# First-layer products of the prologue in fp32, key step on POOL

## The chip, the cores and the metric

The kernel runs on one core of a Trainium2 chip. The metric is the device time of one execution in microseconds; lower is better. Before the change it is 1369.68 us, the median of three runs (1369.66 to 1371.54).

The engines of a core work side by side, each through its own list of instructions in order: PE (TensorE, matrix products, from SBUF into PSUM), DVE (VectorE), ACT (ScalarE), POOL (GpSimd), and SP (SyncE), which here only issues transfers. They meet at semaphores.

## The reference

Three stages follow one another. The first is a gated linear attention over 768 steps for 4 x 8 heads of 48; the second a mixture of four experts, all of them applied, weighed by normalised probabilities; the third a gated two-layer network.

```python
for t in range(S):
    state = alpha[:, :, t, :, None] * state + k[t] (outer) v[t]
    y[:, :, t] = q[t] @ state
x = y as rows of 3072 tokens by 384
p = domain_probs / domain_probs.sum(-1)
out = sum over e of p[:, e] * (relu(x @ w1[e]) @ w2[e])      # 4 experts, 384 -> 1024 -> 384
h = out @ w_in                                               # 384 -> 2048
result = (h * clip(h + 3, 0, 6) / 6) @ w_out                 # 2048 -> 384
```

All inputs and outputs are fp32.

## The kernel before, in words

**Tiles.** The 3072 tokens make 6 tiles of 512. Attention is done in chunks of 64 steps for all heads, 8 chunks to a tile (`PER_TILE`). The two networks are cut into slots: a slot is 128 hidden units, its weights are 384 columns for the first layer and 384 for the second (128x768 together). A tile has 32 slots of the experts and 16 of the third stage.

**Products in two parts.** A product of fp32 operands in the networks is made of three products in a reduced format (fp32r): each operand is split into a high part (a rounded copy, made by ACT) and a low part (the rest). `hidden(g)` is the first layer of slot g (L571 to L589): for each of three blocks of x (`K3`) the products hi*hi, hi*lo and lo*hi, at L587. `project(g)` is the second layer (L591 to L607, product at L606). `weights_hi(g)` (L951 to L955, ACT) and `weights_lo(g)` (L1069 to L1077, POOL) split a slot's weights from the loaded `w_raw`, a ring of 4, into the rings `w_hi` and `w_lo` of 8.

**Attention of a chunk n.** POOL makes the decays and scales k level by level (`scale_k`, steps 0 to 5; the step into `k_top` is L1053). The last step, into `k_level(n, 6)`, is made by ACT for the first eight chunks (`scale_k_last`, L883 to L890, four copies) and by POOL from chunk 8 on (L1048). DVE scales q (`scale_q`, L664 and L680). PE makes the scores (`score`, L498), turns the keys (`turn_k`, L510), and does `attend`: masked scores by v (L540), the new part of the state (`carry`, L520), and q by the state (L555). Between `score` and `attend` DVE masks the scores (`keep`, L697 and L709), with two of the levels copied by ACT (`copy_high`, L905). After `attend` DVE forms the next state (L721) and turns y (L727), ACT writes the high part of x (`split_x`, L930), and DVE the low part (L733). `score(n+2)` writes the PSUM banks that y(n) was in, and so waits for these two parts.

**The prologue.** The first tile's eight chunks are done before the main loop over slots. PE's order is: score(n+1), a warming matmul on zeros (`keep_warm`, L563, 128x256 in fp32), attend(n), turn_k(n+1), and after chunks 4, 5 and 6 two early slots each (`early_after`): the first layer of slots 0 to 5 for the first half of the tile's tokens, the 256 of chunks 0 to 3 (`HALF`). After the early slots 4 and 5 come five warming matmuls, attend(7), four more, and the main loop with slot 0. There, slots 0 to 5 do the second half of the tokens only. ACT splits high parts of slots 0 to 5 in its iterations 0 to 5; POOL low parts of slots 0 to 5 in its iterations 3 to 8 of ten, right after its first k step, in two halves.

**The main loop.** For every slot g PE does `hidden(g)`, then `score`, `turn_k` or `attend` of a chunk of the next tile where tables place them, then `project(g - 2)`. Weights are split three slots ahead and loaded six ahead. SP's queue holds all loads in one order, so a load that waits holds those behind it.

## Time and profile before

| | before |
|---|---|
| median of three runs | 1369.68 us |
| profiled execution | 1370.62 us |
| its span | 1368.8 us |
| PE busy | 1349.2 us (99%) |
| POOL busy | 781.8 us (57%) |
| DVE busy | 653.9 us (48%) |
| ACT busy | 553.6 us (40%) |
| granted PE clock, mean | 0.999 |

The span is the time from the first to the last instruction in the profile; the execution has 1.8 us around it. Busy shares are means over the span. The chain that ended last goes back from the last instruction, at each step to what released it, or to the instruction before it on its engine.

### The profile page before, as it was taken

The numbers are of one execution on the slowest core, as the hardware profiler recorded it, in microseconds if no ns is written. First come the engines' busy times: TensorE is split into PE (matmuls) and PEld (weight loads), VectorE is DVE, ScalarE is ACT, GpSimd is POOL, SyncE is SP. The second block draws the span as 40 slices with busy tenths as digits, with TensorE's granted clock in tenths as the row PEclk, the third lists the DMA queues.
The fourth block names the chain that finished last, engine by engine and source line by source line (L and its number), as shares of the span: only waits on it lengthen the run. The fifth ranks groups of instructions, "written<-read, shape, count | busy, mean of one in ns | idle before, by whom it ended". The sixth has DMA issues, their size and how long they took to land.

```text
span 1368.8 us, 34311 instructions
## 1 busy us (share of the span) xinstructions
PE 1349.2 (99%) x13638; PEld 1104.4 (81%) x13638; DVE 653.9 (48%) x1382; ACT 553.6 (40%) x1078; POOL 781.8 (57%) x862
## 2 busy tenths in 40 slices
PE   7899999999999999999999999999999999999998
PEld 5788888888888888888888888888888888888887
DVE  7756655444544544454544444444445333333333
ACT  5633333333444333355332345433335433335543
POOL 8956665566556565656556555665564444444442
PEclk9999999999999999999999999999999999999999
DMA  5353333333333433333433333343332343323331
GB/s 161 91 169 111 110 110 117 109 117 98 100 123 104 141 99 125 96 107 108 149 105 107 108 107 106 117 129 112 98 97 85 98 127 103 110 93 93 103 116 35
DMA packets 76045, 150.35 MB, mean 110 GB/s; under 512 B 8816, under 2 KB 33648, under 8 KB 75888
## 3 DMA queue, kind: packets, MB, share of 16 engines
q1 hardware_dynamic: 75888, 148.16, 34.2%
q8 instruction: 111, 1.82, 0.6%
q14 instruction: 46, 0.38, 0.1%
HBM read 143.36 MB, written 4.77 MB: 108 GB/s over the span
## 4 chain that ended last, share of the span: by engine, by line
PE 97%; DVE 1%; issue 1%; POOL 0%; DMA 0%; ACT 0%; DVEq 0%; POOLq 0%
PE psum L606 44%; PE psum L587 43%; PE psum L498 5%; PE psum L520 1%; PE psum L540 1%; PE psum L555 1%; PE psum L510 1%; PE psum L563 1%; DMA alpha_q<-qa 0%; DVE q_lev L680 0%; POOL k_lev L1057 0%; DVE result L780 0%; DVE alpha_q L680 0%; DVE alpha_q L664 0%; DVE decay L651 0%
## 5 line engine op out<-in xcount | busy, mean ns | idle before, releaser
L1076 POOL TENSOR_TENSOR w_lo<-w_raw,w_hi 128x768 fp32r<-128x768 f32 (+1 forms) x294 | 532.7, 1813 | 538.4 <-ACT w_hi L955 538.1
L948 ACT ACTIVATE h_hi<-psum 128x512 fp32r<-128x512 f32 (+1 forms) x288 | 171.1, 595 | 613.9 <-DVE psum L741 531.3
L606 PE MATMUL psum<-h_hi,w_hi 128*128 128x512 f32 x855 | 341.0, 399 | 0.2 <-DVE x_lo L776 0.2
L587 PE MATMUL psum<-x_hi,w_hi 128*128 128x512 f32 (+1 forms) x882 | 339.8, 385 | 0.4 <-issue 0.4
L587 PE MATMUL psum<-x_lo,w_hi 128*128 128x512 f32 (+1 forms) x882 | 339.3, 385 | 0.0
L587 PE MATMUL psum<-x_hi,w_lo 128*128 128x512 f32 (+1 forms) x882 | 339.2, 385 | 0.0
L606 PE MATMUL psum<-h_hi,w_lo 128*128 128x512 f32 x855 | 333.7, 390 | 0.0
L606 PE MATMUL psum<-h_lo,w_hi 128*128 128x512 f32 x855 | 333.2, 390 | 0.0
L741 DVE SCALAR_TENSOR_TENSOR psum<-psum,probs 128x512 f32<-128x512 f32 x184 | 128.6, 699 | 353.4 <-PE psum L587 353.3
L955 ACT ACTIVATE w_hi<-w_raw 128x768 fp32r<-128x768 f32 x288 | 241.5, 838 | 0.1
L759 DVE TENSOR_TENSOR h_lo<-psum,h_hi 128x512 fp32r<-128x512 f32 x280 | 192.3, 687 | 61.0 <-ACT h_hi L948 61.0
L587 PEld LDWEIGHTS psum<-x_hi,w_hi 128*128 128x128 f32 x882 | 165.7, 188 | 34.0 <-issue 0.7
L587 PEld LDWEIGHTS psum<-x_hi,w_lo 128*128 128x128 f32 x882 | 165.7, 188 | 33.2
L587 PEld LDWEIGHTS psum<-x_lo,w_hi 128*128 128x128 f32 x882 | 165.7, 188 | 33.1
L606 PEld LDWEIGHTS psum<-h_hi,w_lo 128*128 128x128 f32 x855 | 160.5, 188 | 34.4
L606 PEld LDWEIGHTS psum<-h_hi,w_hi 128*128 128x128 f32 x855 | 160.5, 188 | 34.2 <-issue 0.6
L606 PEld LDWEIGHTS psum<-h_lo,w_hi 128*128 128x128 f32 x855 | 160.7, 188 | 31.1
L747 DVE SCALAR_TENSOR_TENSOR psum<-gate,psum 128x512 f32<-128x512 f32 x96 | 66.8, 696 | 198.7 <-ACT gate L936 198.7
L936 ACT ACTIVATE gate<-psum,three 128x512 f32<-128x512 f32 x96 | 66.3, 691 | 141.6 <-PE psum L587 141.6
L1057 POOL TENSOR_TENSOR k_lev<-k_lev,decay 128x256 f32<-128x256 f32 x144 | 96.0, 667 | 6.8 <-ACT k_lev L880 0.5
L709 DVE COPY_PREDICATED p_kept<-level_sb,psum 128x128 f32<-128x128 int32 x224 | 74.0, 330 | 5.6
L1020 POOL TENSOR_TENSOR decay<-decay 128x64 f32<-128x64 f32 (+3 forms) x184 | 58.7, 319 | 11.9
(71 smaller groups left out, 843.1 us busy)
## 6 DMA issues: line engine op xcount, KB each, us to landing
w_raw<-w SPq DMA_DIRECT2D x288, 384.0 KB, 3.0
alpha_q<-qa SPq DMA_DIRECT2D x48, 256.0 KB, 3.7
k_raw<-kk SPq DMA_DIRECT2D x48, 128.0 KB, 3.5
probs<-prob_scratch SPq DMA_DIRECT2D x24, 256.0 KB, 3.9
v_sb<-v SPq DMA_DIRECT2D x48, 96.0 KB, 3.0
out<-result SPq DMA_DIRECT2D x18, 256.0 KB, 3.9
level_sb<-level SPq DMA_DIRECT2D x1, 80.0 KB, 3.0
ident_sb<-ident SPq DMA_DIRECT2D x1, 64.0 KB, 3.2
```

Source lines behind the costliest of these rows:

```text
L498: mm = pe.matmul(j_out[own(jj), lo:lo + width], k_level(n, l)[own(i), j, :], moving, start=True, stop=True)
L587: mm = pe.matmul(h_bank[g % 2][:, cols], a, x[:, cols], start=k == 0 and i == 0, stop=k == K3 - 1 and i == 2)
L606: mm = pe.matmul(out_bank[k], a, x, start=first and i == 0, stop=(last or g == PLAIN - 1) and i == 2, skip_group_check=ph == 0)
L709: dve.copy_predicated(dst.rearrange("p a (m r x) -> p a m r x", r=2, x=x)[:, :, :, 1, :], mask, s[:, :, at:at + CH // 2].rearrange("p a (m ...
L741: dve.scalar_tensor_tensor(out=h_bank[g % 2][:, :], in0=h_bank[g % 2][:, :], scalar=0.0, in1=probs[:, t % 2, u, :], op0=ALU.max, op1=ALU.m ...
L747: dve.scalar_tensor_tensor(out=h_bank[g % 2][:, :], in0=gate[:, g % 2, :], scalar=6.0, in1=h_bank[g % 2][:, :], op0=ALU.min, op1=ALU.mult) ...
L759: op = dve.tensor_tensor(lo, h_bank[g % 2][:, :], hi, ALU.subtract)
L936: act.activation(gate[:, g % 2, :], h_bank[g % 2][:, :], ACT.Relu, bias=three[:, :]).then_inc(gate_made, 1)
L948: act.activation(h_at(h_hi, x_hi, g)[:, cols], h_bank[g % 2][:, cols], ACT.Relu if g < PLAIN else ACT.Copy).then_inc(hh_made, 1)
L955: act.activation(w_hi[:, g % RING, :], w_raw[:, g % RAW, :], ACT.Copy).then_inc(w_hi_made, 1)
L1057: op = pool.tensor_tensor(b, a, dec.to_broadcast([P, m, 2, x]), ALU.mult)
L1076: op = pool.tensor_tensor(w_lo[:, g % RING, cols], w_raw[:, g % RAW, cols], w_hi[:, g % RING, cols].bitcast(F32), ALU.subtract)
```

## The change

The first layer of the six early slots is no longer done with three reduced products per block, but with one fp32 product per block (`hidden_early`), straight from the loaded weights `w_raw` and from a copy of x in fp32. ACT writes that copy (`keep_x`) for chunks 0 to 3 into `result`, a tile that the prologue doesn't use otherwise. The ring of raw weights is freed for slots 4 and 5 only when the early slot that read it is done (`h_made` in `load_w`), and these two loads stand one iteration later in SP's order. The last key step of the first eight chunks goes from ACT to POOL. In the prologue ACT and POOL split the weights of slots 0 to 4 instead of 0 to 5; POOL does it in its iterations 5 to 9; slot 5 is split in the main loop, at slot 2. `EARLY` stays 6, so the two new loops over `early_after(PER_TILE - 1)` are empty.

```diff
--- before.py
+++ after.py
@@ -40,7 +40,8 @@
 DEEP = 3
 BEHIND = 2
 PLAIN = FT
-EARLY = 6
+EARLY = 2 * DEEP
+SPLIT_EARLY = 5
 EARLY_FROM = PER_TILE // 2
 HALF = TILE // 2
 SPLIT_AHEAD = 3
@@ -52,7 +53,6 @@
 Z_STEPS = LEVELS - 1
 Z_FIRST = 2
 K_STEPS = 6
-K_SCALES = 4
 KEEPS = LEVELS
 HIGHS = 6
 K_TOP = PAIRS * CH + CH // 2
@@ -143,11 +143,6 @@
 
 def last_of_seq(n):
     return n % SEQ_CH == SEQ_CH - 1
-
-
-def scaled(n):
-
-    return K_STEPS * n - min(n, PER_TILE)
 
 
 def keeps(n):
@@ -236,7 +231,7 @@
         in_prob_rows, prob_rows_out, prob_made = sem("in_prob_rows"), sem("prob_rows_out"), sem("prob_made")
         zeros_made, ones_made, p_zeroed = sem("zeros_made"), sem("ones_made"), sem("p_zeroed")
         three_made = sem("three_made")
-        q_made, k_made, k_last_made = sem("q_made"), sem("k_made"), sem("k_last_made")
+        q_made, k_made = sem("q_made"), sem("k_made")
         z_made, z_first_made, total_made = sem("z_made"), sem("z_first_made"), sem("total_made")
         k_odd_made = sem("k_odd_made")
         p_made, kt_made = sem("p_made"), sem("kt_made")
@@ -244,7 +239,7 @@
         keep_made, high_made, kn_made, dec_made, s_made = sem("keep_made"), sem("high_made"), sem("kn_made"), sem("dec_made"), sem("s_made")
         yt_made, x_hi_made, x_lo_made = sem("yt_made"), sem("x_hi_made"), sem("x_lo_made")
         w_hi_made, w_lo_made = sem("w_hi_made"), sem("w_lo_made")
-        h_made, gate_made, h_out, out_weighed = sem("h_made"), sem("gate_made"), sem("h_out"), sem("out_weighed")
+        h_made, gate_made, h_out, out_weighed, x_kept_made = sem("h_made"), sem("gate_made"), sem("h_out"), sem("out_weighed"), sem("x_kept_made")
         hh_made, hl_made = sem("hh_made"), sem("hl_made")
         out_made, x2_hi_made, out_free = sem("out_made"), sem("x2_hi_made"), sem("out_free")
         stored = sem("stored")
@@ -404,6 +399,7 @@
 
                 need(sp, w_hi_made, g - RAW + 1)
                 need(sp, w_lo_made, g - RAW + 1)
+                need(sp, h_made, min(g - RAW + 1, EARLY))
                 u = PHASE_OF[g]
                 f = g - STARTS[u] + (0 if PHASES[u][0] == "E" else E_SLOTS)
                 sp.dma_start(w_raw[:, g % RAW, :], w[f]).then_inc(in_w[g % RAW], 16)
@@ -436,12 +432,12 @@
                 load_qk(n + QRING)
                 if n > 0:
                     load_v(n + 1)
-                if RAW <= n < LOAD_AHEAD:
-                    load_w(n)
+                if RAW < n <= EARLY:
+                    load_w(n - 1)
             load_v(PER_TILE + 1)
             sp.dma_start(prob_rows[:, :, :], dp.rearrange("e (p n) -> p e n", p=P)).then_inc(in_prob_rows, 16)
             for g in range(SLOTS):
-                if g + LOAD_AHEAD < SLOTS:
+                if EARLY <= g + LOAD_AHEAD < SLOTS:
                     load_w(g + LOAD_AHEAD)
                 if g in SCORE_AT and SCORE_AT[g] + QRING < CHUNKS:
                     load_qk(SCORE_AT[g] + QRING)
@@ -476,7 +472,7 @@
                 pe.wait_ge(in_k[n % QRING], 16 * (n // QRING + 1))
                 pe.wait_ge(k_odd_made, n + 1)
                 pe.wait_ge(q_made, Q_STEPS * n + LEVELS)
-                pe.wait_ge(k_made, scaled(n) + LEVELS - 1)
+                pe.wait_ge(k_made, K_STEPS * n + LEVELS - 1)
                 for l in range(LEVELS):
                     at, width = ((0, CH // 2), (CH // 2, CH))[l] if l < 2 else (CH // 2 * (l + 1), CH // 2)
                     for jp in range(2):
@@ -503,8 +499,7 @@
 
                 if n == 0:
                     pe.wait_ge(in_ident, 16)
-                pe.wait_ge(k_made, scaled(n + 1))
-                pe.wait_ge(k_last_made, K_SCALES * min(n + 1, PER_TILE))
+                pe.wait_ge(k_made, K_STEPS * (n + 1))
                 need(pe, kn_made, carried(n))
                 for jp in range(2):
                     mm = pe.transpose(kt_out[:, jp * P:(jp + 1) * P], k_level(n, LEVELS)[:, 2 * jp:2 * jp + 2, :],
@@ -562,22 +557,30 @@
                 for _ in range(n):
                     pe.matmul(out_bank[2][:, 0:2 * P], zeros_sb[:, 0:P], zeros_sb[:, :], start=True, stop=True)
 
-            def hidden(g, early=False):
+            def hidden_early(g):
+
+                pe.wait_ge(x_kept_made, EARLY_FROM)
+                need(pe, hh_made, made(g, early=True) - 2)
+                need(pe, hl_made, made(g, early=True) - 2)
+                pe.wait_ge(in_w[g % RAW], 16 * (g // RAW + 1))
+                for k in range(K3):
+                    mm = pe.matmul(h_bank[g % 2][:, 0:HALF], w_raw[:, g % RAW, k * P:(k + 1) * P], result[:, k, 0:HALF],
+                                   start=k == 0, stop=k == K3 - 1)
+                mm.then_inc(h_made, 1)
+
+            def hidden(g):
 
                 kind, t = PHASES[PHASE_OF[g]]
-                first = g == STARTS[PHASE_OF[g]] and not early
-                cols = columns_of(g, early)
-                if early:
-                    pe.wait_ge(x_hi_made, EARLY_FROM)
-                    pe.wait_ge(x_lo_made, EARLY_FROM)
+                first = g == STARTS[PHASE_OF[g]]
+                cols = columns_of(g)
                 if first and kind == "E":
                     pe.wait_ge(x_hi_made, PER_TILE * (t + 1))
                     pe.wait_ge(x_lo_made, PER_TILE * (t + 1))
                 if first and kind == "M":
                     pe.wait_ge(x2_hi_made, K3 * (t + 1))
                     pe.wait_ge(out_free, K3 * (PHASES.index(("E", t)) + 1))
-                need(pe, hh_made, made(g, early) - 2)
-                need(pe, hl_made, made(g, early) - 2)
+                pe.wait_ge(hh_made, made(g) - 2)
+                pe.wait_ge(hl_made, made(g) - 2)
                 pe.wait_ge(w_hi_made, g + 1)
                 pe.wait_ge(w_lo_made, g + 1)
                 for k in range(K3):
@@ -623,7 +626,7 @@
                     if not early_after(n):
                         keep_warm(1)
                 for g in early_after(n):
-                    hidden(g, early=True)
+                    hidden_early(g)
             for g in range(SLOTS):
                 hidden(g)
                 if g in SCORE_AT:
@@ -837,6 +840,8 @@
                 split_x(n)
                 if not last:
                     scale_q(ahead, at + behind + 1)
+            for g in early_after(PER_TILE - 1):
+                hidden_lo(g, early=True)
             for step in range(Q_EARLY):
                 scale_q(Q_BEFORE, step)
             for g in range(SLOTS):
@@ -879,16 +884,6 @@
                 a, b = (k_level(n, l).rearrange("p j (m r) -> p j m r", r=2)[:, :, :, 1] for l in (0, 1))
                 act.activation(b, a, ACT.Copy).then_inc(k_odd_made, 1)
 
-            def scale_k_last(n):
-
-                wait_decays(act, n, LEVELS - 1)
-                act.wait_ge(k_made, scaled(n) + LEVELS - 1)
-                need(act, kt_made, carried(n - 1))
-                dec = decay_k(n, LEVELS - 1)
-                for j in range(PAIRS):
-                    act.activation(k_level(n, LEVELS)[:, j, 0:CH // 2], k_level(n, LEVELS - 1)[:, j, 0:CH // 2],
-                                   ACT.Copy, scale=dec[:, j, 0:1]).then_inc(k_last_made, 1)
-
             def copy_high(n):
 
                 s = scores(n)[:, :].rearrange("p (a c) -> p a c", c=SLAB)
@@ -919,6 +914,13 @@
                     act.activation(state_decayed[:, j, :], state[n % 2][:, j, :], ACT.Copy,
                                    scale=total[n % 2][:, j:j + 1]).then_inc(dec_made, 1)
 
+            def keep_x(n):
+
+                act.wait_ge(yt_made, n + 1)
+                cols = slice(n * CH, (n + 1) * CH)
+                act.activation(result[:, :, cols].rearrange("p b (h t) -> p b h t", h=2), y_blocks(n), ACT.Copy
+                               ).then_inc(x_kept_made, 1)
+
             def split_x(n):
 
                 t = n // PER_TILE
@@ -966,9 +968,7 @@
             odd_k(0)
             odd_k(1)
             odd_k(2)
-            scale_k_last(0)
             copy_high(0)
-            scale_k_last(1)
             for n in range(PER_TILE):
                 copy_k_rows(n)
                 for g in early_after(n - 1):
@@ -979,11 +979,13 @@
                     odd_k(n + 3)
                 if n + 1 < PER_TILE:
                     copy_high(n + 1)
-                if n < EARLY:
+                if n < SPLIT_EARLY:
                     weights_hi(n)
+                if n < EARLY_FROM:
+                    keep_x(n)
                 split_x(n)
-                if n + 2 < PER_TILE:
-                    scale_k_last(n + 2)
+            for g in early_after(PER_TILE - 1):
+                hidden_hi(g, early=True)
             for g in range(SLOTS):
                 if g > BEHIND and g - BEHIND in STARTS and PHASES[PHASE_OF[g - BEHIND - 1]][0] == "E":
                     x2_hi(PHASE_OF[g - BEHIND - 1])
@@ -992,7 +994,7 @@
                 hidden_hi(g)
                 if g in STATE_AT:
                     split_x(STATE_AT[g])
-                if EARLY <= g + SPLIT_AHEAD < SLOTS:
+                if SPLIT_EARLY <= g + SPLIT_AHEAD < SLOTS:
                     weights_hi(g + SPLIT_AHEAD)
                 if g in SCORE_AT:
                     n = SCORE_AT[g]
@@ -1014,8 +1016,6 @@
                     need(pool, q_made, Q_STEPS * (n - 1))
                 else:
                     wait_decays(pool, n, l - 1)
-                if l == LEVELS - 1:
-                    need(pool, k_last_made, K_SCALES * min(n - 1, PER_TILE))
                 first, second = decay_operands(n, l)
                 pool.tensor_tensor(decay_pair(n, l), first, second, ALU.mult).then_inc(z_made, 1)
 
@@ -1042,7 +1042,7 @@
                     wait_decays(pool, n, l)
                 if l == LEVELS - 2:
                     need(pool, kt_made, carried(n - 1))
-                pool.wait_ge(k_made, scaled(n) + l)
+                pool.wait_ge(k_made, K_STEPS * n + l)
                 if l == LEVELS - 1:
                     dec = decay_k(n, l)[:, :, 0:1].to_broadcast([P, PAIRS, x])
                     op = pool.tensor_tensor(k_level(n, l + 1)[:, :, 0:x], k_level(n, l)[:, :, 0:x], dec, ALU.mult)
@@ -1085,15 +1085,14 @@
                 pool.memset(p_kept[i][:, :, :, :], 0.0).then_inc(p_zeroed, 1)
             for n in range(K_BEFORE):
                 for l in range(K_STEPS):
-                    if l < LEVELS - 1 or n >= PER_TILE:
-                        scale_k(n, l)
-                    if l == 0 and 0 <= n - K_BEFORE + EARLY + 1 < EARLY:
-                        weights_lo(n - K_BEFORE + EARLY + 1, 2)
+                    scale_k(n, l)
+                    if l == 0 and n >= K_BEFORE - SPLIT_EARLY:
+                        weights_lo(n - K_BEFORE + SPLIT_EARLY, 2)
                     if l < Z_STEPS and Z_FIRST <= n + 1 < K_BEFORE:
                         decays(n + 1, l + 1)
                 decay_all(n)
             for g in range(SLOTS):
-                if EARLY <= g + SPLIT_AHEAD < SLOTS:
+                if SPLIT_EARLY <= g + SPLIT_AHEAD < SLOTS:
                     weights_lo(g + SPLIT_AHEAD)
                 if g in K_AT:
                     n, a, b = K_AT[g]
```

## Rows read from the trace of the kernel before

**Rows 1.** The page: span, busy time by engine, and the chain's shares.
```profile
span 1368.8 us, 34311 instructions
PE 1349.2 (99%) x13638; PEld 1104.4 (81%) x13638; DVE 653.9 (48%) x1382; ACT 553.6 (40%) x1078; POOL 781.8 (57%) x862
...
PE 97%; DVE 1%; issue 1%; POOL 0%; DMA 0%; ACT 0%; DVEq 0%; POOLq 0%
```

**Rows 2.** The chain of waits, prologue: start us, duration us, what.
```profile
45.53 2.15 PE psum L587 x18
...
51.72 2.23 PE psum L587 x18
...
57.41 1.25 issue
...
61.87 2.16 PE psum L563 x10
...
65.07 1.92 PE psum L563 x8
```

**Rows 3.** Timeline of PE: start us, us, line, operation, count, idle before and releaser.
```profile
12.99 0.66 PE L510 MATMUL psum<-ident_sb,k_top 128*128 128x128 f32 x2 [1.43 <-ACT k_top L889]
...
23.99 0.41 PE L540 MATMUL psum<-v_sb,p_kept 64*32 64x48 f32 x32 [0.57 <-issue]
...
33.20 0.43 PE L498 MATMUL psum<-alpha_q,k_raw 64*64 64x32 f32 x16 [0.42 <-DVE x_lo L733]
...
50.24 0.40 PE L540 MATMUL psum<-v_sb,p_kept 64*32 64x48 f32 x32 [0.32 <-issue]
...
54.01 0.43 PE L498 MATMUL psum<-alpha_q,k_raw 64*64 64x32 f32 x16
...
56.65 0.40 PE L540 MATMUL psum<-v_sb,p_kept 64*32 64x48 f32 x32
...
63.96 0.40 PE L540 MATMUL psum<-v_sb,p_kept 64*32 64x48 f32 x32
...
66.82 0.36 PE L587 MATMUL psum<-x_hi,w_hi 128*128 128x256 f32 x1
```

**Rows 4.** Timeline of POOL, prologue.
```profile
19.54 2.14 POOL L1076 TENSOR_TENSOR w_lo<-w_raw,w_hi 128x384 fp32r<-128x384 f32 x2
21.97 0.44 POOL L1020 TENSOR_TENSOR decay<-alpha_q 128x128 f32<-128x128 f32 x1 [0.29 <-DVE q_lev L680]
...
53.25 0.62 POOL L1053 TENSOR_TENSOR k_top<-k_lev,decay 128x256 f32<-128x256 f32 x1
...
60.59 0.40 POOL L1048 TENSOR_TENSOR k_top<-k_top,decay 128x128 f32<-128x128 f32 x1
```

**Rows 5.** Timeline of DVE, prologue.
```profile
19.65 1.17 DVE L680 TENSOR_TENSOR q_lev<-q_lev,decay 128x256 f32<-128x256 f32 x1
...
25.83 0.46 DVE L680 TENSOR_TENSOR q_lev<-q_lev,decay 128x256 f32<-128x256 f32 x1
...
28.30 0.88 DVE L664 TENSOR_TENSOR alpha_q<-alpha_q,decay 128x128 f32<-128x128 f32 x1
...
54.17 0.32 DVE L664 TENSOR_TENSOR alpha_q<-alpha_q,decay 128x128 f32<-128x128 f32 x1
...
60.87 0.74 DVE L697 COPY_PREDICATED p_kept<-diag_sb,psum 128x256 f32<-128x256 int32 x1
...
62.66 0.62 DVE L709 COPY_PREDICATED p_kept<-level_sb,psum 128x128 f32<-128x128 int32 x2
```

**Rows 6.** Timeline of ACT, prologue.
```profile
11.90 0.94 ACT L889 ACTIVATE k_top<-k_top,decay 128x32 f32<-128x32 f32 x4
...
25.95 0.33 ACT L930 ACTIVATE x_hi<-psum 128x192 fp32r<-128x192 f32 x1 [0.45 <-DVE psum L727]
```

**Rows 7.** The page's DMA issues: engine, count, KB each, us to landing.
```profile
w_raw<-w SPq DMA_DIRECT2D x288, 384.0 KB, 3.0
```

**Rows 8.** Windows: stretch, us, busy time by engine (PE first), PEclk, DMA, GB/s.
```profile
38.00:41.00 3.00, 3.00 (x38) 2.06 (x42) 2.96 (x8) 1.27 (x6) 3.00 (x9) 0.50 0.36 85
```


## The prediction

> **What bounds the kernel now.** I read the page first. The span is 1368.8 us, TensorE is busy for 1349.2 us of it and carries 97% of the chain that ended last [rows 1]. About 1,300 us of this is the main loop, in which TensorE runs without pause at the full clock; the diff leaves its products as they are, and only moves the split of one weight slot (slot 5) into its first slots. So the change can act only in the prologue, which ends where the first product of the main loop starts, at 66.82 us [rows 3]. The question is by how much that instant moves; the rest of the span moves with it. Of the prologue I then read the chain of waits, in order of time [rows 2], and each engine's timeline [rows 3 to 6].
>
> The reader should see three regimes. (a) Up to the attend of chunk 1, TensorE is mostly held by its own order. (b) For chunks 2 to 5 a loop through VectorE sets the pace: masking of chunk n, attend(n), state, turn, high part on ScalarE, low part on VectorE, masking of chunk n+1. The signs are score(4), which waited for a low part of x [rows 3], and the idle of TensorE ahead of attend(1) and attend(5) [rows 3]. POOL runs without pause beside it and is the second limit: the 128x256 step that ends its work for score(7) starts at 53.25 and takes 0.62 [rows 4], and score(7) starts at 54.01 [rows 3]. (c) From attend(5) at 50.24 to 66.82 TensorE is held by its own order nearly all the time: turn of the keys, a pair of early slots (2.23 us), score(7), attend(6) at 56.65, an unexplained pause of 1.25 us, the next pair, ten warming rows (2.16 us), attend(7) at 63.96, eight more (1.92 us) [rows 2, 3].
>
> **The change, part by part.**
>
> *Early products in fp32.* A pair of early slots is 18 one-pass products now and costs 2.15 to 2.23 us on the chain, three times [rows 2]. After, a slot is three fp32 products of 128x256. The warming matmul has that very shape and type, and one of it shows as two rows; ten rows took 2.16 us and eight 1.92 us [rows 2], so 0.216 to 0.24 each. A pair becomes 12 rows: 2.59 to 2.88 us. Less the 2.15 to 2.23 of now, that is +0.36 to +0.73 a pair; I take +0.42, since the longer row of warming stands nearer to an unbroken pair. Three pairs make +1.3 us of work. The pairs of regime (c), after attend(5) and attend(6), have nothing to hide behind: +0.84. The pair ahead of score(6) had 0.32 us of TensorE idle behind it [rows 3], so it costs at most 0.1 by itself, but it uses up what VectorE may gain in between. The Trainium skill says the same in "FP8 and Floating Point Precision" (TensorE Precision Notes), four passes for true fp32; twelve passes against nine would by that rule add a third to a pair, some 0.7 us; with that for all three pairs the sum would be 0.9 us higher than mine.
>
> *Low parts later on POOL.* Now POOL splits one slot per iteration in iterations 3 to 8, as two instructions, 2.14 us for the first [rows 4]. After, iterations 5 to 9 do it. Iterations 3 and 4 lose 2.1 us each, iteration 9 gains it, and slot 5 is split in the main loop. Two effects. First, POOL's own order: iteration 3 gains nothing by it, because its next decay waits for the q steps of chunk 2 in any case (it began at 21.97, released by VectorE [rows 4]). Second, VectorE runs faster where POOL is quiet: a 128x128 product of two SBUF tiles took 0.32 us alone and 0.88 beside a low part, and the 128x256 q step of chunk 0 took 1.17 against 0.46 [rows 5]. That is 0.6 to 0.7 us a time. Followed through: the q step at 19.65 ends 0.7 earlier, and attend(1) comes 0.55 earlier, capped by the 0.57 of idle ahead of it [rows 3]; masking of chunk 2 loses another collision, about 0.6. From chunk 3 on the low parts are back, at about the same point of the loop, so nothing more is gained.
>
> *A copy of x on ScalarE* for chunks 0 to 3, ahead of the high part. No row shows an fp32 copy of this shape; the nearest is the high part itself, same shape and source, 0.33 us [rows 6]. Pipelined behind each other such copies can start 0.1 closer, so 0.23 to 0.33; I take 0.25. For chunk 1 VectorE waits for the high part (it started at 25.95, released by the turn [rows 6], and the low part came right behind it), so there and in chunk 2 the copy lies on the loop, +0.25 each. In chunk 0 and 3 a q step covers it to about 0.1. For chunks 4 to 7 nothing is added.
>
> Loop balance at attend(2): 0.55 + 0.6 less 0.25 is 0.85 earlier (some 0.05 goes elsewhere); at score(4), after the second copy, 0.65 earlier. It stays at 0.65 over chunks 3 and 4.
>
> *Last key step back on POOL.* It costs 0.40 us (the same step of chunk 8 [rows 4]) and frees ScalarE of four copies, 0.94 us a chunk [rows 6]. It is eight steps, 3.2 us of POOL, against one slot less to split in the prologue, 2.1. Chunk 0: ScalarE no longer holds the first turn of the keys (1.43 us of TensorE idle [rows 3]), but score(1) waits for POOL's k_top, and attend(0) follows it in order, so nothing of it remains. POOL meets score(5) to score(7) with two splits less (4.2) and up to seven steps more (2.8), less what iteration 3 could not use: about 1.3 earlier at score(5), shrinking by 0.36 a chunk to about 0.9 at score(7). So POOL is no longer what score(7) waits for; it could have started 0.9 earlier, but TensorE's pair ahead of it is not done.
>
> *Waits.* The loads of slots 4 and 5 now wait for h_made too, that is for the first pair of early slots. Behind each in SP's queue stands the load of chunk 10 or 11, which waits for later scores in any case. A load lands in 3.0 us [rows 7]; issued at about 46 and 52 us it is there at 56 at the latest, and the pair that needs it starts at about 59. Nothing for ScalarE, POOL or SP ends later than its use.
>
> *Main loop.* Slot 4's low part is made at about 61 to 63.5 us, ahead of the main loop, and slot 5's right behind its high part in slot 2, at about 74 to 76 by the order of ScalarE; the products that need them come in slots 4 and 5, with an attend, scores and projections of earlier slots between. SP's load of slot 9 waits for the latter, three slots ahead of its split. I put the cost at nothing; should hidden(5) wait all the same, it is at most one low part, 2.1 us.
>
> **The sum.** attend(4) comes 0.65 earlier. Then the first pair, +0.42, makes TensorE the one that is late at attend(5): 0.65 less 0.42 plus the idle of 0.32 that it fills leaves attend(5) 0.55 earlier. From there on TensorE's own order holds all, with two pairs: -0.55 + 0.84 is +0.3 us at 66.82. Against the profiled execution, 1370.62 us (span 1368.8 and 1.8 around it), that is 1370.9. The median of the three runs shown is 0.94 below the profiled execution; on that footing it is 1370.0.
>
> **Rivals.**
> 1. *Forecast*: gain in the VectorE loop and loss in the fp32 pairs cancel, 1370.0. For it: regime (c) is fixed by order and its warming matmuls stay. Chance 0.62.
> 2. *The pause goes.* The 1.25 us inside the carry of chunk 6 [rows 2] belongs to no data wait. If other instructions ahead of it remove it, 1368.8; with the clock fall of rival 3 gone as well, at most 0.5 less. Against: nothing in the diff aims at it, and the loads of chunk 11 are issued just before it as they are now. Chance 0.12.
> 3. *TensorE's clock.* After the idle ahead of attend(3) the granted clock was 0.50, the 1.2 GHz level, over at least 3 us [rows 8], a loss of 1.5 us of work that the VectorE loop mostly hid. If the fall shifts into regime (c), it is on the chain: +1.5, 1371.5. Chance 0.09.
> 4. *Slower: POOL's lock.* Every POOL step that reads SBUF can hold a VectorE product of two SBUF tiles, as the rows of 0.88 against 0.32 show. There are eight more such steps of 0.40, and the split of slot 4 (2.1) now falls beside the masking of chunk 7, which starts at 60.87 [rows 5]. If all of the eight fall on the loop and the relief of 0.65 is eaten: 0.3 + 3.2 is 1373.2. It decides from the point where the delays pass the 0.7 us that VectorE has in hand ahead of attend(7) (its masking ended at 63.28 by the last row, attend(7) started 0.68 later). Against: most masking steps read PSUM, and two splits of 2.1 us leave the same stretch. The skill's "SBUF — State Buffer" (Who interferes with whom) calls the shared pair an exclusive lock for the whole instruction, which speaks against this change; the trace agrees with the lock, not with its always being hit. Half of it, +1 us (1371.0), has chance 0.10, all of it 0.05.
> 5. *The change hits nothing*, the early slots being bound by the new waits on loads: then the pair after attend(6) starts late, by 1 us at most, 1371. Chance 0.02.
>
> **Chances and range.** Faster by over 0.2% (2.7 us, about what a measurement of this kernel can tell from no change) needs the pause, the clock fall and a longer gain together: 0.04, out of the 0.12 of rival 2. Slower by over 0.2%: rival 4 in full, 0.05, and 0.01 of rival 3 for a clock fall twice as long, 0.06 together. Same: 0.90. The range takes in rival 2 at the bottom and rivals 3 and the half of 4 at the top: 1368.3 to 1371.9.
>
> **What would show it.** In the profile of the changed kernel: the first product of the main loop starts at 67.1 instead of 66.8; the pairs take 2.6 to 2.9 us as 12 rows; attend(1) to attend(5) come 0.5 to 0.9 earlier and this lead is gone by attend(6); POOL has idle ahead of score(7) or ends its step for it near 53; the q steps of chunks 0 and 2 lose their 0.9 and 1.17 us forms; ScalarE has four more 0.33 copies and 32 fewer key copies. The prediction is wrong if pauses of TensorE without a data wait appear or vanish by over 1 us, if the low clock lands after 50 us, or if the main loop's own length changes at all.

## The result and the profile after

The changed kernel takes 1377.22 us (median of 6 runs, 1376.44 to 1379.03) against 1369.7 us for the kernel before (6 runs): the ratio is 1.0051, with a 95% interval of 1.0038 to 1.0064. It is slower by 7.5 us; the forecast was 1370.0, in a range up to 1371.9.

| | before | after |
|---|---|---|
| median | 1369.7 us | 1377.2 us |
| profiled execution | 1370.62 us | 1379.03 us |
| its span | 1368.8 us | 1377.2 us |
| PE busy | 1349.2 us | 1352.4 us |
| PE idle in the span | 19.6 us | 24.8 us |

The page of the kernel after, in the order of rows 1, and then two of its groups of instructions (line, engine, operation, count | busy, mean ns | idle before, releaser).

```profile
span 1377.2 us, 34196 instructions
...
PE 1352.4 (98%) x13620; PEld 1105.9 (80%) x13620; DVE 653.0 (47%) x1382; ACT 547.7 (40%) x1050; POOL 782.4 (57%) x869
...
PE 96%; POOL 1%; issue 1%; DVE 1%; DMA 0%; ACT 0%; DVEq 0%; POOLq 0%; ACTq 0%; SPq 0%
...
L957 ACT ACTIVATE w_hi<-w_raw 128x768 fp32r<-128x768 f32 x288 | 241.5, 838 | 6.2 <-DMA w_raw<-w 6.1
```

The last line is the first hint. The 288 splits of weights on ScalarE cost what they did, but one idle time of 6.1 us stands ahead of them, and a load ended it. The timeline of PE after shows what that did (to be read beside [rows 3]).

```profile
24.59 0.40 PE L535 MATMUL psum<-v_sb,p_kept 64*32 64x48 f32 x32
...
44.31 0.41 PE L535 MATMUL psum<-v_sb,p_kept 64*32 64x48 f32 x32 [0.91 <-issue]
...
46.07 2.76 PE L567 MATMUL psum<-result,w_raw 128*128 128x256 f32 x12
52.48 0.43 PE L494 MATMUL psum<-alpha_q,k_raw 64*64 64x32 f32 x16 [3.65 <-ACT x_hi L932]
...
56.08 0.58 PE L535 MATMUL psum<-v_sb,p_kept 64*32 64x48 f32 x32 [0.96 <-issue]
...
58.18 4.15 PE L567 MATMUL psum<-result,w_raw 128*128 128x256 f32 x12
62.26 0.43 PE L494 MATMUL psum<-alpha_q,k_raw 64*64 64x32 f32 x16
...
74.00 0.36 PE L590 MATMUL psum<-x_hi,w_hi 128*128 128x256 f32 x1
```

The same two places in the timeline of PE before, the pair's first product and score(6):

```profile
45.29 0.36 PE L587 MATMUL psum<-x_hi,w_hi 128*128 128x256 f32 x1
...
47.61 0.43 PE L498 MATMUL psum<-alpha_q,k_raw 64*64 64x32 f32 x16
```

After, score(6) starts 6.4 us after the first pair of early slots began, with 3.65 us of idle ahead of it; before, it was 2.3 us after. The next pair takes 4.15 us and not 2.76 as the first. The main loop starts at 74.00 instead of 66.82. The timeline of ACT, and below it that of SP's queue, tell why score(6) had to wait.

```profile
43.12 1.50 ACT L900 ACTIVATE p_kept<-psum 32x128 f32<-32x128 f32 x6
50.72 0.84 ACT L957 ACTIVATE w_hi<-w_raw 128x768 fp32r<-128x768 f32 x1 [6.10 <-DMA w_raw<-w]
51.59 0.33 ACT L932 ACTIVATE x_hi<-psum 128x192 fp32r<-128x192 f32 x1
51.81 0.38 ACT L907 ACTIVATE k_rows<-psum 128x256 f32<-128x256 f32 x1
```

```profile
47.64 0.33 SPq L405 DMA_DIRECT2D w_raw<-w  x1
```

ScalarE comes to the high part of slot 4's weights at 44.6 us, right after its copies of the top levels of chunk 5. The load of slot 4 now waits for the first early slot to be done, since that slot reads the same buffer; it is issued at 47.64 and lands at 50.7. In all this time the high part of x of chunk 4 stands behind in ScalarE's queue, though y(4) was turned at 46.6. score(6) needs it, so TensorE stands too. After its idle the clock falls, not at once: the rows of score(6) still take the short time, 0.43 us for sixteen, and the granted clock is low in the windows behind it (columns as in rows 8):

```profile
53.00:56.00 3.00, 2.12 (x79) 1.49 (x70) 3.00 (x10) 2.23 (x10) 3.00 (x7) 0.70 0.18 57
56.00:59.00 3.00, 2.92 (x84) 2.45 (x84) 1.87 (x5) 0.43 (x2) 3.00 (x8) 0.50 0.30 96
```

The span grew by 8.4 us. Its parts, from the two profiles: 0.8 before the first pair begins (45.29 to 46.07); 6.4 from there to the main loop (21.5 us before, 27.9 after); and 1.2 for a pause in the main loop, at score(9), that has no data wait. The profiled execution is the slowest of the six, 1.8 us above their median, so the pause need not be in the others:

```profile
84.98 1.23 issue
```

### The profile page after: what moved, and what is told of

Its sections match the earlier page's. It is cut to its first block, busy times and chain, and to the rows that moved or that the text cites. A ratio compares the mean times of both kernels' runs of the same rounds, so it can differ in the third digit from the quotient of the medians.

```text
span 1377.2 us, 34196 instructions
## 1 busy us (share of the span) xinstructions
PE 1352.4 (98%) x13620; PEld 1105.9 (80%) x13620; DVE 653.0 (47%) x1382; ACT 547.7 (40%) x1050; POOL 782.4 (57%) x869
## 4 chain that ended last, share of the span: by engine, by line
PE 96%; POOL 1%; issue 1%; DVE 1%; DMA 0%; ACT 0%; DVEq 0%; POOLq 0%; ACTq 0%; SPq 0%
PE psum L609 43%; PE psum L590 42%; PE psum L494 5%; PE psum L535 1%; PE psum L515 1%; PE psum L505 1%; PE psum L550 1%; PE psum L558 1%; PE psum L567 1%; POOL k_lev L1057 0%; DMA alpha_q<-qa 0%; POOL decay L1020 0%; DMA w_raw<-w 0%; DVE q_lev L683 0%; POOL k_top L1053 0%
## 5 line engine op out<-in xcount | busy, mean ns | idle before, releaser
L590 PE MATMUL psum<-x_hi,w_hi 128*128 128x512 f32 (+1 forms) x864 | 334.5, 387 | 0.0
L590 PE MATMUL psum<-x_hi,w_lo 128*128 128x512 f32 (+1 forms) x864 | 334.1, 387 | 0.3 <-issue 0.3
L590 PE MATMUL psum<-x_lo,w_hi 128*128 128x512 f32 (+1 forms) x864 | 334.2, 387 | 0.0
L590 PEld LDWEIGHTS psum<-x_hi,w_hi 128*128 128x128 f32 x864 | 162.2, 188 | 33.9 <-issue 0.8
L590 PEld LDWEIGHTS psum<-x_lo,w_hi 128*128 128x128 f32 x864 | 162.2, 188 | 33.3
L590 PEld LDWEIGHTS psum<-x_hi,w_lo 128*128 128x128 f32 x864 | 162.2, 188 | 33.1
```

What stands on the lines that cost most here:

```text
L590: mm = pe.matmul(h_bank[g % 2][:, cols], a, x[:, cols], start=k == 0 and i == 0, stop=k == K3 - 1 and i == 2)
```

## The experiments

**Theory A**: ScalarE stands at the wait for slot 4's load with the high part of x(4) queued behind it, TensorE idles, and the clock falls. **Theory B**: POOL has too much, by the eight last key steps and their lock on VectorE. **Theory C**: the fp32 products cost more than their rows say.

**1. The step moved out of the way.** A small edit in the changed kernel (between the two places stands what is not changed).

```diff
-                if n < SPLIT_EARLY:
+                if n < EARLY_FROM:
                     weights_hi(n)
...
                 split_x(n)
+                if n == EARLY_FROM + 1:
+                    weights_hi(EARLY_FROM)
```

> The changed kernel, with one step of ScalarE moved: the high part of slot 4's weights is made in iteration 5, behind the high part of x of chunk 5, not in iteration 4 ahead of that of chunk 4. Theory A (ScalarE stood at the wait for slot 4's load, which waits for the first early slot, with the high part of x(4) queued behind; the idle of TensorE that followed also brought the clock down): the stall of about 4.8 us and the low clock after it, about 2.4 us, both go; time about 1370 to 1372, that is within 2 us of the kernel before, and score(6) starts 2.7 us after the pair's start, not 6.4. Theory B (POOL has too much: eight last key steps and their lock on VectorE): no more than 1 us of change, about 1376 to 1377. Theory C (the fp32 pairs): no change, 1377.

Measured: 1370.50 us (10 runs), ratio to before 0.9999 (0.9990 to 1.0009). All of the loss is gone. Its timeline of PE:

```profile
45.15 2.76 PE L567 MATMUL psum<-result,w_raw 128*128 128x256 f32 x12
...
47.83 0.44 PE L494 MATMUL psum<-alpha_q,k_raw 64*64 64x32 f32 x16
...
58.40 0.36 PE L550 MATMUL psum<-state,q_lev 64*32 64x48 f32 x21 [0.69 <-issue]
...
66.67 0.35 PE L590 MATMUL psum<-x_hi,w_hi 128*128 128x256 f32 x1
```

score(6) follows the pair without idle, and the main loop begins at 66.67, 0.15 us earlier than before the change. Everything else of the change is in this kernel, so theories B and C fall as causes of the loss.

**2. The same cause taken away at its other end.** Five buffers for raw weights: slot 4 has a buffer of its own, and its load waits for no early slot.

```diff
-RAW = 4
+RAW = 5
```

> The changed kernel with five buffers for raw weights instead of four, so that slot 4's load does not wait for an early slot; ScalarE's order is as in the changed kernel. Theory A: the same gain as by moving the step, 1370 to 1372, since the load is there long before ScalarE asks for it. If instead ScalarE's order as such cost the time (the 0.84 us split ahead of the high part of x), at most 1 us is gained here. Theories B and C: 1376 to 1377.

Measured: 1370.45 us (10 runs), ratio 0.9998 (0.9989 to 1.0007). ScalarE's order is that of the changed kernel, so the split ahead of the high part of x costs nothing that the medians show. It is the late load in that place.

**3. The stall kept, the idle filled.** How much of the loss is the stall, and how much the clock?

```diff
                 for g in early_after(n):
                     hidden_early(g)
+                if n == EARLY_FROM:
+                    keep_warm(10)
```

> The changed kernel with ten warming matmuls (20 rows, about 4.4 us) after the first pair of early slots, in the stretch in which TensorE stood idle. The stall stays, the idle goes. Theory A: score(6) starts at about the same time as in the changed kernel (within 0.5 us), the granted clock stays at 1.00 over the next 6 us, and the second pair takes 2.7 us and not 4.15; in all about 2.4 us are gained, 1374.5 to 1375.5. If the low clock cost nothing beyond the stall: 1377.

Measured: 1373.41 us (10 runs), ratio 1.0021 (1.0012 to 1.0030). That is 3.8 us less than the changed kernel, more than the 2.4 that I expected. PE's timeline, and the window in which the changed kernel had 0.50:

```profile
44.70 2.76 PE L567 MATMUL psum<-result,w_raw 128*128 128x256 f32 x12
...
51.70 0.43 PE L494 MATMUL psum<-alpha_q,k_raw 64*64 64x32 f32 x16
...
55.18 2.75 PE L567 MATMUL psum<-result,w_raw 128*128 128x256 f32 x12
...
69.59 0.35 PE L590 MATMUL psum<-x_hi,w_hi 128*128 128x256 f32 x1
```

```profile
56.00:59.00 3.00, 3.00 (x86) 2.49 (x88) 2.84 (x7) 1.91 (x8) 3.00 (x6) 1.00 0.59 193
```

From the first pair to the main loop it takes 24.9 us: 3.4 more than the 21.5 of experiment 1, which is the stall, and 3.0 less than the 27.9 of the changed kernel, which is the clock. The split is a little unfair to the clock, for the filling is longer than the stall. ACT and the added products in this run:

```profile
50.35 0.33 ACT L934 ACTIVATE x_hi<-psum 128x192 fp32r<-128x192 f32 x1
```

```profile
47.30 4.48 PE L558 MATMUL psum<-zeros_sb 128*128 128x256 f32 x20
```

In the changed kernel score(6) came 0.9 us after the start of this high part (51.59 and 52.48). By that it could have come at about 51.2 here (my estimate), and it came at 51.70, right behind the last added product. So some 0.5 us of the 3.4 belongs to the filling, and the clock cost 3.0 to 3.5 us. Warming products that compute nothing gained 3.8 us by the medians, since nearly all of them ran in time that was lost anyway.

**4. The last key step alone.** The kernel before with `scale_k_last` removed from ScalarE and all six steps of the first eight chunks on POOL.

```diff
-                    if l < LEVELS - 1 or n >= PER_TILE:
-                        scale_k(n, l)
+                    scale_k(n, l)
```

> The kernel before with one part of the change alone: the last key step of the first eight chunks on POOL; early products, splits and loads as before. It prices the lock and the load of POOL by themselves. Theory A needs it small: 8 x 0.40 us more on POOL, which was the limit for score(7) only: +0.4 to +2.5 us, 1370 to 1372. Theory B: +5 us or more, 1375 or above.

Measured: 1371.44 us (10 runs) against 1370.11 for the kernel before in the same comparison; the ratio of the record, 0.9999 (0.9990 to 1.0009), does not tell them apart, though the medians lie 1.3 us apart. POOL's added work does show as idle of TensorE where the low parts are still early:

```profile
40.95 0.43 PE L498 MATMUL psum<-alpha_q,k_raw 64*64 64x32 f32 x16 [2.29 <-POOL k_top L1046]
...
55.42 0.43 PE L498 MATMUL psum<-alpha_q,k_raw 64*64 64x32 f32 x16 [1.50 <-POOL k_top L1046]
...
67.15 0.35 PE L586 MATMUL psum<-x_hi,w_hi 128*128 128x256 f32 x1
```

score(5) and score(7) wait for POOL. The first wait is hidden by others (attend(4) is not later than before), the second is not: attend(6) starts at 57.58, 0.9 us later than before. The main loop starts only 0.33 us later, because the pause without a data wait in chunk 6, 1.25 us before [rows 2], lasts 0.66 us in this profile. Theory B would have needed 5.

**5. The gate alone.** The kernel before with the later loads, and one step of ScalarE moved with them: the high part of slot 5 comes one iteration later. The first condition of the main loop's loads changes as in the diff of the change, and is left out here.

```diff
                 need(sp, w_lo_made, g - RAW + 1)
+                need(sp, h_made, min(g - RAW + 1, EARLY))
...
-                if RAW <= n < LOAD_AHEAD:
-                    load_w(n)
+                if RAW < n <= EARLY:
+                    load_w(n - 1)
...
-                if n < EARLY:
+                if n <= EARLY_FROM:
                     weights_hi(n)
+                if n == EARLY_FROM + 2:
+                    weights_hi(EARLY_FROM + 1)
```

> The kernel before with the gate alone: the loads of slots 4 and 5 wait for the first and second early slot and stand one iteration later, as in the changed kernel; early products, key step and low parts as before; only the high part of slot 5 is made one iteration later on ScalarE, so that slot 4's is the only one that stands ahead of a late load. Theory A: the load of slot 4 is issued at about 46.5 us, lands 3 to 4 us later, its high part and then that of x(4) follow, and score(6) starts at 51.5 to 52.5 us instead of 47.6; with the low clock after the idle that makes 1374.5 to 1378. If the loss belonged to another part of the change: within 1 us of the kernel before.

Measured: 1375.69 us (4 runs), ratio 1.0045 (1.0031 to 1.0058). Its timelines of ACT and of PE:

```profile
49.46 0.84 ACT L956 ACTIVATE w_hi<-w_raw 128x768 fp32r<-128x768 f32 x1 [5.61 <-DMA w_raw<-w]
50.33 0.33 ACT L931 ACTIVATE x_hi<-psum 128x192 fp32r<-128x192 f32 x1
```

```profile
44.90 0.36 PE L588 MATMUL psum<-x_hi,w_hi 128*128 128x256 f32 x1
...
51.22 0.65 PE L499 MATMUL psum<-alpha_q,k_raw 64*64 64x32 f32 x16 [3.93 <-ACT x_hi L931]
...
67.12 0.35 PE L588 MATMUL psum<-x_hi,w_hi 128*128 128x256 f32 x1 [1.73 <-POOL w_lo L1079]
```

From the pair's first product to score(6) it is 6.3 us, as in the changed kernel (6.4). The stall is reproduced with reduced products, the key step on ScalarE and early low parts. The last line is a side effect of my own edit (slot 5's parts were made later, and the early products need them here); so the 6.0 us of this kernel aren't the gate's price alone.

**6. The fp32 products alone.** The kernel before with `hidden_early` and `keep_x`, and five raw buffers (the two functions themselves and the wait in `load_w`, both as in the change, are left out).

```diff
+RAW = 5
...
                 for g in early_after(n):
-                    hidden(g, early=True)
+                    hidden_early(g)
...
+                if n < EARLY_FROM:
+                    keep_x(n)
                 split_x(n)
```

> The kernel before with the fp32 early products and the fp32 copy of x alone, and five buffers for raw weights, so that no load ScalarE waits for is late; key step on ScalarE and splits as before. My sum: +0.4 us for each of two pairs on the chain, +0.25 for each of two copies, hidden or not by the loop: 1370 to 1372, pairs of 2.6 us. If fp32 products cost more than their rows say: above 1372.5.

Measured: 1370.81 us (10 runs), ratio 1.0007 (0.9998 to 1.0016); within what the sum gives. In the profiled execution the second pair met the low clock:

```profile
44.73 2.76 PE L573 MATMUL psum<-result,w_raw 128*128 128x256 f32 x12
...
50.93 0.40 PE L541 MATMUL psum<-v_sb,p_kept 64*32 64x48 f32 x32 [1.28 <-issue]
...
52.55 4.08 PE L573 MATMUL psum<-result,w_raw 128*128 128x256 f32 x12
```

No load was late here, and the idle ahead of attend(5) was 1.28 us. So this fall of the clock, my rival 3 as it was meant, can come without the stall; the main loop of this execution starts at 68.31, 1.5 us later than before.

**7 and 8. The smallest edit, twice.** The high part of slot 4's weights right behind that of x(4), in the same iteration.

```diff
-                if n < SPLIT_EARLY:
+                if n < EARLY_FROM:
                     weights_hi(n)
...
                 split_x(n)
+                if n == EARLY_FROM:
+                    weights_hi(EARLY_FROM)
```

> The changed kernel with the smallest edit: on ScalarE the high part of slot 4's weights stands right behind that of x(4), not ahead of it. ScalarE still stands at the load until about 49.5 to 50.5 us, but what is queued behind is now the copy of the turned keys of chunk 5 and the copies of the top levels of chunk 6. Theory A: score(6) starts right behind the pair (2.7 us after its start); attend(5) is late by 0.3 to 1.5 us, in all 1370.5 to 1372.5. If any wait of ScalarE at that load cost the full stall: 1375 or above.

Measured: 1373.90 us (6 runs), ratio 1.0033 (1.0021 to 1.0045), from 1369.42 to 1376.51. I expected at most 1372.5. The profiled execution was the fastest; so the kernel ran again.

> The same kernel as the one with the high part of slot 4 right behind that of x(4), once more, for another profile and more executions. Again a spread of over 4 us; in a slow execution the profile would show a granted clock of 0.50 somewhere between 45 and 60 us (theory of the clock), or a high part of slot 4 that starts later than 50 us with the clock at 1.00 (theory of the load).

Measured: 1374.85 us (10 runs, 1373.54 to 1377.18), ratio 1.0032 (1.0022 to 1.0042). The two profiles, that of experiment 7 first; for each SP's queue and ACT, and for the second PE and a window as well:

```profile
45.40 0.33 SPq L405 DMA_DIRECT2D w_raw<-w  x1
...
48.40 0.84 ACT L957 ACTIVATE w_hi<-w_raw 128x768 fp32r<-128x768 f32 x1 [3.59 <-DMA w_raw<-w]
```

```profile
46.17 0.33 SPq L405 DMA_DIRECT2D w_raw<-w  x1
...
51.32 0.84 ACT L957 ACTIVATE w_hi<-w_raw 128x768 fp32r<-128x768 f32 x1 [5.82 <-DMA w_raw<-w]
...
52.81 0.58 PE L535 MATMUL psum<-v_sb,p_kept 64*32 64x48 f32 x32 [3.29 <-issue]
54.91 4.91 PE L567 MATMUL psum<-result,w_raw 128*128 128x256 f32 x12
...
56.00:59.00 3.00, 3.00 (x8) 2.38 (x8) 2.96 (x9) 0.47 (x2) 2.71 (x5) 0.50 0.43 134
```

The same load takes 3.0 us from issue to ScalarE's start in one execution and 5.15 in the other. In the four other profiles in which ScalarE stood at it (the changed kernel, experiments 3, 5 and 9) it takes 3.05 to 3.2. What stands behind ScalarE's wait now is the copy of the turned keys of chunk 5, which attend(5) needs. After 3.0 us attend(5) waits 0.98 us, half a microsecond more than in experiment 1; after 5.15 it waits 3.29 us and the clock falls. From the first pair to the main loop it takes 21.9 us in the one and 26.8 in the other, which is 4.9 of the 5.9 us between the two executions. So the stall is not gone: it falls on the next user in ScalarE's queue, and the clock multiplies what is left.

**9. Is that spread the clock or the load?** The kernel of 7 with two warming matmuls more ahead of attend(4) and of attend(5).

```diff
-                keep_warm(1 if n + 1 < PER_TILE else 5)
+                keep_warm(5 if n + 1 == PER_TILE else 3 if n in (4, 5) else 1)
```

> The kernel with the high part of slot 4 right behind that of x(4) spread over 7 us, 1369.4 to 1376.5. Here it has two warming matmuls more (0.86 us) ahead of attend(4) and attend(5), where TensorE idled 1.12 and 0.98 us in its profile. If the spread is TensorE's clock, which falls in some executions after that idle: median 1370 to 1371.5 and a spread of at most 3 us. If it is the landing time of slot 4's load, on which ScalarE still stands: the spread stays at 5 us or more.

Measured: 1373.72 us (10 runs, 1370.35 to 1376.94), ratio 1.0021 (1.0009 to 1.0033). The spread stays at 6.6 us and the median does not fall to 1370 or 1371.5, so a clock that falls after those two idles is not the cause. That it is the load, my other theory, is not shown by this run. Its profiled execution (1372.59 us) against the fast one of experiment 7 (1369.42 us), the first pair of each, experiment 7 first, and then ScalarE here:

```profile
43.83 2.75 PE L567 MATMUL psum<-result,w_raw 128*128 128x256 f32 x12
```

```profile
46.80 2.76 PE L567 MATMUL psum<-result,w_raw 128*128 128x256 f32 x12
```

```profile
51.43 0.84 ACT L957 ACTIVATE w_hi<-w_raw 128x768 fp32r<-128x768 f32 x1 [3.65 <-DMA w_raw<-w]
```

The load was issued at 48.38 and took 3.05 us, yet the first pair began 3.0 us later, nearly the whole 3.2 us between the two; 2.1 us of that stand at attend(1) already (25.40 against 23.32), ahead of the added matmuls. So a part of the spread arises ahead of the load. The kernel before, too, had one execution of 29 at 1376.48 us in the same comparison. The load's landing time is shown for one slow execution, the profiled one of experiment 8. How much of the spread it makes, and why it varies, is open.

**10 and 11. Two tries for a kernel that beats both.** First the kernel of experiment 1 with three warming matmuls instead of five ahead of attend(7).

```diff
-                keep_warm(1 if n + 1 < PER_TILE else 5)
+                keep_warm(1 if n + 1 < PER_TILE else 3)
```

> The changed kernel with the high part of slot 4 made in iteration 5, and three warming matmuls instead of five ahead of attend(7). A try for a kernel that beats both: in the run with five, masking of chunk 7 was over before the warming ended. Expected: attend(7) 0.4 to 0.9 us earlier and the clock still at 1.00; 1369 to 1370. If masking is what ends last: no change, 1370.4.

Measured: 1370.21 us (11 runs), ratio 1.0002 (0.9993 to 1.0011). In its profile attend(7) comes at 61.99 and the main loop at 64.84, 2 us earlier than before the change, but that execution, 1368.5 us, was the fastest of the eleven; the median shows nothing of it. Then one warming matmul more ahead of attend(3) to attend(5), against falls of the clock.

> A second try for a kernel that beats both: the high part of slot 4 in iteration 5, three warming matmuls ahead of attend(7), and one more ahead of attend(3), attend(4) and attend(5), where TensorE idles 0.4 to 1.1 us. If falls of the clock in some executions are what keeps the median of the two earlier kernels up: 1368.8 to 1369.8, and a spread under 2 us. If not: 1370.2 as with three warming matmuls alone.

Measured: 1370.97 us (12 runs), ratio 1.0002 (0.9992 to 1.0011). No gain either. No version beat the kernel before.

## Why the prediction was wrong, step by step

**The step that failed** is the paragraph on waits: "Nothing for ScalarE, POOL or SP ends later than its use." I worked out when the load of slot 4 is issued (about 46 us) and lands (3.0 us later, about 49) and compared it with the early pair that needs it, at 59 us. I did not compare it with its first reader. That is ScalarE's split of the same weights in its iteration 4. The timelines of ACT and of SP's queue before have the split and the load that it reads:

```profile
44.17 0.84 ACT L955 ACTIVATE w_hi<-w_raw 128x768 fp32r<-128x768 f32 x1
```

```profile
38.48 0.89 SPq L409 DMA_DIRECT2D w_raw<-w  x1
```

With the new wait the load can't be there before 49, some 5 us after ScalarE asks for it. I named what stands behind the load in SP's queue, and not what stands behind the reader in ScalarE's: the high part of x(4), on which score(6) waits. In place of the nothing that the sum had for this wait, the profiles show 3.65 us of idle, then 3.0 us or a little more at the low clock. Experiment 1 moves that reader and recovers 6.7 us by the medians; experiment 2 moves the load and recovers as much; experiment 5 puts the gate into the old kernel and makes the stall. The Trainium skill has the rule that makes such a wait dear, in "TensorE: Matmul & The Clock Gate" (Architectural detail), where it calls ScalarE's and VectorE's queues strict first-in first-out; the trace agrees: x_hi starts right after the split it had no need of (50.72 and 51.59).

**The clock**, my rival 3: right in kind, wrong in size and in its trigger. I had 1.5 us for a fall that shifts into the last stretch. It came, behind an idle that I had not foreseen, and cost 3.0 to 3.5 us by the profiles (experiment 3), because it lay on the chain for longer: attend(5) ran wholly at the 1.2 GHz level (granted clock 0.50), and the second pair, 4.15 us for 2.76, for the most part (0.50, then 0.67 in the next 3 us).

**The fp32 pairs**: right. 12 rows, 2.59 us on the chain of waits in experiment 1, the lower end of my 2.59 to 2.88. I had also named the four passes of true fp32 in the Trainium skill, "FP8 and Floating Point Precision" (TensorE Precision Notes): a third more for a pair, 2.9 to 3.0 by my estimate. The trace shows less: a reduced product took 0.12 us, and an fp32 product, two rows, 0.43, about 3.5 times as much. What the rows are in passes no run shows.

**The copy of x**: right. 0.33 us, 0.23 from its start to that of the high part behind it (40.06 and 40.29 in the timeline of ACT after).

**The last key step**: right in its price, 0.40 us. By experiment 4 its effect alone is at most about 1.3 us, and with the low parts later it is less: in the changed kernel score(5) and score(7) don't wait for POOL.

**Low parts later**: half right. The q step of chunk 0 went from 1.17 to 0.77, not to 0.46. attend(1) came 0.6 us later in the profile of the changed kernel and 0.6 earlier in that of experiment 3; the difference is score(2), whose first sixteen rows took 0.65 us in the one and 0.43 in the other. The lead of 0.65 at attend(4) did not appear: 43.38 in experiment 1 and 43.22 in experiment 3, against 43.36 before. Where the two gains went no run tells. (The prediction's own steps give 0.60 and not 0.65, 0.85 less the second copy's 0.25.)

**The sum without the stall**: 0.3 us at the main loop's start was forecast; -0.15 (experiment 1) and +0.4 (experiment 2, 67.21) were measured. That is near, but in part by luck. attend(5) was to come 0.55 us earlier and came 0.3 later in experiment 1 (50.53 against 50.24) and 0.8 later in experiment 2. What made up for it, in the main, is the pause without a data wait in chunk 6, which my sum kept at 1.25 us and which lasts 0.69 and 0.72 us in these profiles. So the times show that these parts of the change cost next to nothing together; that a gain in VectorE's loop pays for the fp32 pairs is not shown. The time of this case is made by one wait that the sum had at nothing.

**Rival 4** (POOL's lock) got 0.15, and no run shows it. The rival that happened, a late load ahead of ScalarE's queue, was not on my list; rival 5 came nearest, with 0.02, but for the wrong reader.

The pause of 1.23 us at score(9) in the main loop is in the one profile of the changed kernel. No run tells its cause.

## What to carry to other kernels

When a load gets a new wait, list all readers of its buffer, and begin with the one that comes first on any engine, also if it is not the reader that the change is about. For that reader, write down what is queued behind it: the price is not the delay of the reader but that of the next instruction with a user on the chain. And if TensorE will idle for some microseconds in any case, products on zeros there can keep the clock for what follows (3.8 us in experiment 3), as long as they end before the wait does. Against idles of about 1 us they gained nothing here (experiments 9 and 11).

## What the runs showed of the hardware

- After an idle of 3.65 us on TensorE the granted clock went to 0.50, some 2 us after the engine was busy again, and a pair of 12 rows took 4.15 us instead of 2.76; in all the low clock cost about as much as the stall itself (3.0 us beside 3.4 us). With the idle filled the clock stayed at 1.00 (experiment 3). Idles of 3.93 and 3.29 us (experiments 5 and 8) had a fall with them too.
- Shorter idles are not so clear: 1.28 us in experiment 6 had a fall behind it, and 1.34 us ahead of attend(3) had one before the change [rows 8] and none at the same place in experiment 3.
- One load of 384 KB took 3.0 us in one execution and 5.15 in another of the same kernel, and 3.05 to 3.2 in four profiles of others. The kernel's time spread over 7 us (1369.42 to 1376.51); only a part of that is traced to the load.
- An fp32 product of 128x256 cost 1.16 times the three reduced products that it replaces (2.59 us against 2.23 for a pair of slots).
